# Re-timed steps in the attention plan of a fused attention and two-MLP kernel: natural keys of chunk 2, GpSimd's products of block 0, masks of chunk 5

## The chip, the cores and the metric

The kernel runs on one core of one Trainium2 chip. The metric is the device time of one execution in microseconds (us), lower is better. The kernel before takes 418.03 us, the median of 3 runs (417.99 to 418.68).

## The reference

Three layers follow one another, all in 32-bit floating point. Only the first and the routing part of the third matter for the change.

```python
# 1. attention with a decaying state: B, H, S, D = 2, 8, 768, 48
for t in range(S):
    cur = einsum('bhd,bhe->bhde', u * k[t], v[t])
    y[:, :, t] = einsum('bhd,bhde->bhe', r[t], state + cur)
    state = w * state + einsum('bhd,bhe->bhde', k[t], v[t])
# 2. x = y as 1536 tokens x 384; h = x @ w_in (384 x 2048); x2 = elu(h) @ w_out
# 3. logits = x2 @ w_gate (8 experts); expert = argmax; gate = softmax probability of it
#    each token takes the next of its expert's 384 places, goes through
#    relu(x2 @ w1[e]) @ w2[e], and comes back times its gate
```

## The kernel before

**Chunks, blocks, steps.** The 1536 tokens are 12 chunks of 128; six chunks make one batch element, and within it the attention state is carried from chunk to chunk. Two chunks make a block of 256 tokens for the first MLP, so there are six blocks (n = 0 to 5). A block has 16 steps (f = 0 to 15), one for each 128 of the 2048 hidden features. Steps are counted through: step q = 16 n + f, so block 0 is steps 0 to 15 and block 1 is steps 16 to 31. Chunks 0 and 1 are computed before step 0. The attention of chunks 2 to 11 is spread over the MLP's steps, as small pieces on each engine.

**A step on each engine.** Each product is made of three matmuls from a high and a low part of both operands.
- TensorE: fc1(f) (L1475), nine matmuls of 256 columns; then the attention pieces of the step; then, in block 1 and later, the routing's count (L1564) where it is due; then fc2 of three steps ago (L1501), six matmuls. fc1 of step q waits until VectorE has finished the elu of step q-2 (its PSUM bank is free then). fc2 of a step waits for that step's g_lo.
- ScalarE: in block 0 relu(-h) (L861), which waits for g_lo of step q-2, since that frees the elu buffer; exp (L863); a weight cast; the cast g_hi (L872).
- VectorE: from block 1 on min(h, 0) (L1179); the elu itself (L1187); and after it the step's attention pieces and the routing. In block 0 two weight splits of 128x384 a step (wd_lo, L1057 and L1062), one ahead of the elu and one behind it.
- GpSimd: g_lo = elu - g_hi (L707), then the step's attention pieces, by `ahead` (L687).

**The attention pieces of a chunk c.** GpSimd makes the decayed keys and queries (`keys` L638, `queries` L644), the bonus product r*k (`raw_bonus` L602) times u (`with_u` L611), the decayed natural keys (`natural_k1` L616, tile nat, 128x512), and the diagonal (`diagonal` L626, two selects). VectorE sums the bonus (`sum_bonus` L1015) and masks the scores in two halves (`mask` L1020). TensorE makes the scores (L1363), the outer product of natural keys and values (`outer` L1394, which waits for the natural keys), and the result (`back` L1411).

**What sets the order.** Every engine runs its own queue in order. `meeting(c)` and `plan(c)` (L330 to L354) say by hand in which step each piece of a chunk is issued: meeting is 2, 9, 17, 22 and 29 for chunks 2 to 6. An engine asks `chunk_for(what, n, f)` (L358) in every step. In `ahead` the diagonal comes first, then the decay, then natural keys, keys, queries, rk, with_u. On VectorE the masks stand ahead of the routing pieces of the same step.

With the kernel before, the pieces that the change speaks of stand as follows.
- GpSimd, block 0: step 2 diagonal(2) and decay; step 3 natural(2) and keys(3); step 4 queries(3); step 5 rk(3); step 6 with_u(3); step 7 diagonal(3); step 8 natural(3); step 9 nothing.
- VectorE: mask(2, second half) in step 7, ahead of the sum of chunk 3's bonus; mask(5) in steps 23 and 24.
- TensorE: outer(2) in step 9, behind scores(3) and ahead of back(2) and fc2 of step 6. outer(3) is in step 13.

**The routing of block 0's tokens** (`route(0)`, L319) runs in block 1 on VectorE: shift in step 23 (L1098: a copy of 128x8, a maximum, a subtraction), choose in step 24 (L1113: key L1115, maximum L1117, onehot L1118, the sum `before` L1119, n_seen L1121), gates in step 25 (L1123: a sum L1126, a scalar add L1127, a reciprocal L1128, a copy L1129, a product L1130, a sum L1131), place in step 27. Each operation waits for the one before it. TensorE's count of step 26 waits for L1119. On GpSimd steps 23 to 26 carry keys(6), queries(6), rk(6) and with_u(6).

```python
def fc1(n, f):
    q = FT * n + f
    wait_if(pe, s_g, q - 1)
...
def count(n):
    pe.wait_ge(s_round, 2)
    pe.wait_ge(s_oh, n + 1)
...
def outer(c):
    pe.wait_ge(s_k1n, n_states(c + 1))
```

Of the kernel before, what the change touches and what calls it, by code (L numbers as in the profile page):

```python
# [12 lines left out]
def build(nc, B, H, S, D, DFF, NE, FE, CAP, rkt_in, nat_in, decay, bonus, bonus_pair, win, wout, wouttr, wgate, wexp, out, slots):  # L13
# [163 lines left out]
    with ctx:  # L177
# [152 lines left out]
        def meeting(c):  # L330

            return {2: 2, 3: 9, 4: FT + 1, 5: FT + 6, 6: 2 * FT - 3}.get(c, 2 * FT + 3 + 8 * (c - 7))

        def plan(c):

            b, before = meeting(c), meeting(c - 1)
            steps = {"scores": b, "decay": b + (2 if c > 4 else 0), "keys": before + 1, "queries": before + 2,
                     "mask0": b + (c > 4), "mask1": b + 1 + (c > 4)}
            if c == 2:
                steps.update(diagonal=2, mask0=4, mask1=7, natural=3, outer=9, back=9, state=10, low=11)  # L340
                del steps["keys"], steps["queries"]
            elif c < 5:
                steps.update(rk=before + 3, with_u=before + 4, sum=before + 5, diagonal=before + 5, natural=before + 6)
                if c == 3:
                    steps.update(decay=12, outer=13, back=13, low=13, state=14)
            else:
                steps.update(rk=b - 2, with_u=b - 1, sum=b, diagonal=b, natural=b + 4)
            if c == 6:
                steps.update(rk=b - 4, with_u=b - 3)
            if c == 7:  # L350
                steps.update(rk=b - 3)
            if c > 3:
                steps.update(outer=meeting(c + 1), state=meeting(c + 1), back=meeting(c + 1), low=meeting(c + 1))
            return steps  # L354

        PLANS = {c: plan(c) for c in range(2, NSTEP)}

        def chunk_for(what, n, f):  # L358
# [1505 lines left out]
```

## Time and profile before

| | |
|---|---|
| median of 3 runs | 418.03 us (417.99 to 418.68) |
| the profiled execution | 418.21 us, its span 416.5 us |
| TensorE busy | 407.3 us, 98% |
| VectorE busy | 243.5 us, 58% |
| ScalarE busy | 188.0 us, 45% |
| GpSimd busy | 231.8 us, 56% |
| mean granted TensorE clock | 0.997 |

The span is what the profiler sees between the first and the last instruction; the time is 1.7 us longer. Engines in the rows below: PE is TensorE, PEld its weight loads, DVE VectorE, ACT ScalarE, POOL GpSimd. A row of a timeline gives the start in us from the span's start, the duration in us, the engine, the line, the operation, the tiles and the shapes. "x1" is one instruction. In square brackets stands how long the engine was idle before it and what ended that. Matmuls are pipelined: a 256-column matmul is shown with 0.28 us, and the next one starts 0.12 us later.

### The profile page before, as it was taken

The page shows a single profiled execution, that of the slowest core. Times are in us where ns is not written, and L with a number is a line of the kernel's source. Part 1 is how long each engine was busy: PE and PEld are TensorE (multiplying, and loading weights), DVE is VectorE, ACT ScalarE, POOL GpSimd, SP SyncE. Part 2 cuts the span into 40 slices and gives each one's busy share as a digit, 9 for nine tenths or more (in the row PEclk, how much of TensorE's full clock was granted, in tenths as well). Part 3 has the DMA queues.
Part 4 walks back from the last instruction along what each step waited for, and adds up shares of the span by engine and source line. Part 5 has one row for each costly group of instructions (what it writes and reads, how often), then busy time and mean ns, then how long its engine had stood idle before and what let it go on. Part 6 is the DMA issues. An engine that isn't in the chain of part 4 may idle for free.

```text
span 416.5 us, 9128 instructions
## 1 busy us (share of the span) xinstructions
PE 407.3 (98%) x3537; PEld 391.2 (94%) x3537; DVE 243.5 (58%) x576; ACT 188.0 (45%) x409; POOL 231.8 (56%) x239
## 2 busy tenths in 40 slices
PE   8999999999999999999999999999999999999994
PEld 7798799999999999999999999999999999999994
DVE  7788754376567546754663487785535545364521
ACT  4777453223433343334343455553646445574520
POOL 3789856557865786578334335166083562826531
PEclk9999999999999999999999999999999999999998
DMA  7998997123130403020009001826373835739000
GB/s 258 400 395 347 321 373 279 35 83 102 56 118 0 139 19 120 2 87 19 3 2 357 3 0 40 312 89 221 150 302 89 352 136 227 275 102 358 7 33 28
DMA packets 18649, 64.97 MB, mean 156 GB/s; under 512 B 2203, under 2 KB 11717, under 8 KB 16432
## 3 DMA queue, kind: packets, MB, share of 16 engines
q1 hardware_dynamic: 16816, 59.68, 39.2%
q0 software_dynamic: 1792, 4.73, 3.0%
q8 instruction: 27, 0.44, 0.4%
q14 instruction: 14, 0.11, 0.1%
HBM read 51.98 MB, written 13.21 MB: 157 GB/s over the span
## 4 chain that ended last, share of the span: by engine, by line
PE 90%; DVE 3%; POOL 2%; issue 2%; DMA 1%; ACT 0%; SPq 0%; POOLq 0%; DVEq 0%; ACTq 0%
PE bank L1359 26%; PE bank L1361 25%; PE bank L1360 25%; PE bank L1377 2%; DMA rkt<-rkt 1%; PE bank L1406 1%; PE bank L1442 1%; PE bank L1446 1%; PE bank L1680 1%; PE bank L1435 1%; POOL g_lo L707 1%; PE bank L1438 1%; DVE wd_lo L1057 1%; PE bank L1533 1%; PE bank L1715 1%
## 5 line engine op out<-in xcount | busy, mean ns | idle before, releaser
L707 POOL TENSOR_TENSOR g_lo<-elu,g_hi 128x256 fp32r<-128x256 f32 x95 | 73.7, 777 | 88.4 <-ACT g_hi L872 88.2
L1359 PE MATMUL bank<-xt,wd_hi 128*128 128x256 f32 x285 | 80.8, 284 | 0.5 <-DVE elu L1187 0.3
L1361 PE MATMUL bank<-xt,wd_lo 128*128 128x256 f32 x285 | 80.5, 282 | 0.0
L1360 PE MATMUL bank<-xt,wd_hi 128*128 128x256 f32 x285 | 80.4, 282 | 0.0
L863 ACT ACTIVATE elu<-elu 128x256 f32<-128x256 f32 x96 | 40.1, 418 | 77.0 <-DVE elu L1179 76.5
L1359 PE MATMUL bank<-wd_hi,g_hi 128*128 128x392 f32 (+1 forms) x192 | 67.6, 352 | 0.2 <-POOL g_lo L707 0.2
L1187 DVE SCALAR_TENSOR_TENSOR elu<-elu,bank 128x256 f32<-128x256 f32 x96 | 40.3, 419 | 43.7 <-ACT elu L863 43.7
L1361 PE MATMUL bank<-wd_hi,g_lo 128*128 128x392 f32 (+1 forms) x192 | 65.2, 340 | 0.0
L1360 PE MATMUL bank<-wd_lo,g_hi 128*128 128x392 f32 (+1 forms) x192 | 65.2, 339 | 0.0
L872 ACT CAST g_hi<-elu 128x256 fp32r<-128x256 f32 x96 | 39.0, 406 | 42.9 <-DVE elu L1187 42.9
L1359 PEld LDWEIGHTS bank<-xt,wd_hi 128*128 128x128 f32 x285 | 54.0, 189 | 1.6 <-DVE elu L1187 1.5
L1361 PEld LDWEIGHTS bank<-xt,wd_lo 128*128 128x128 f32 x285 | 54.2, 190 | 0.0
L1360 PEld LDWEIGHTS bank<-xt,wd_hi 128*128 128x128 f32 x285 | 54.0, 190 | 0.0
L1291 DVE SCALAR_TENSOR_TENSOR ge_lo<-bank,ge_hi 128x256 fp32r<-128x256 f32 x56 | 23.8, 424 | 48.8 <-ACT ge_hi L930 48.8
L1179 DVE TENSOR_SCALAR elu<-bank 128x256 f32<-128x256 f32 x80 | 33.8, 422 | 31.4 <-PE bank L1361 26.8
L930 ACT ACTIVATE ge_hi<-bank 128x256 fp32r<-128x256 f32 x56 | 21.6, 385 | 54.5 <-PE bank L1361 32.5
L724 POOL TENSOR_TENSOR wd_lo<-wd_raw,wd_hi 128x1024 fp32r<-128x1024 f32 x12 | 30.4, 2560 | 26.6 <-ACT wd_hi L943 24.2
L1359 PEld LDWEIGHTS bank<-wd_hi,g_hi 128*128 128x128 f32 x192 | 36.3, 189 | 3.4 <-issue 2.4
L1360 PEld LDWEIGHTS bank<-wd_lo,g_hi 128*128 128x128 f32 x192 | 36.5, 190 | 0.0
L724 POOL TENSOR_TENSOR we_lo<-we_raw,we_hi 128x1024 fp32r<-128x1024 f32 x9 | 21.3, 2398 | 27.1 <-ACT we_hi L943 27.1
L1361 PEld LDWEIGHTS bank<-wd_hi,g_lo 128*128 128x128 f32 x192 | 36.1, 188 | 0.0
L729 POOL DMA_INDIRECT out<-yrow,tok_i x16 | 15.7, 983 | 18.6 <-DVE yrow L1311 11.7
(220 smaller groups left out, 946.9 us busy)
## 6 DMA issues: line engine op xcount, KB each, us to landing
we_raw<-wexp SPq DMA_DIRECT2D x8, 1536.0 KB, 7.0
wd_raw<-wexp SPq DMA_DIRECT2D x8, 1536.0 KB, 6.7
rkt<-rkt SPq DMA_DIRECT2D x12, 512.0 KB, 5.6
nat<-nat SPq DMA_DIRECT2D x9, 672.0 KB, 4.3
xrow<-slots SPq DMA_DIRECT2D x16, 193.0 KB, 7.0
wd_raw<-win SPq DMA_DIRECT2D x4, 768.0 KB, 9.3
wd_raw<-wout SPq DMA_DIRECT2D x4, 768.0 KB, 9.5
wo_tr<-wouttr SPq DMA_DIRECT2D x1, 3072.0 KB, 18.6
```

The lines of the kernel that those rows point to most:

```text
L707: nc.gpsimd.tensor_tensor(g_lo[:, f % 4, :], elu[:, f % 2, :], g_hi[:, f % 4, :].bitcast(F32), ALU.subtract).then_inc(s_glo, 1)
L724: nc.gpsimd.tensor_tensor(EL[r][:, cols], ER[r][:, cols], EH[r][:, cols].bitcast(F32), ALU.subtract).then_inc(s_elo2[r], 1)
L729: nc.gpsimd.indirect_dma_start(out=out, out_offset=bass.IndirectOffsetOnAxis(ap=tok_i[r][:, t, :], axis=0), in_=yrow[r][:, t, :], in_offse ...
L863: nc.scalar.activation(elu[:, f % 2, :], elu[:, f % 2, :], ACT.Exp, scale=-1.0 if n == 0 else 1.0).then_inc(s_exp, 1)
L872: nc.scalar.copy(g_hi[:, f % 4, :], elu[:, f % 2, :]).then_inc(s_ghi, 1)
L930: nc.scalar.activation(ge_hi[:, f % 4, :], ps_e[f % 2][:, 0:SN], ACT.Relu).then_inc(s_gehi, 1)
L1179: V.tensor_scalar_min(elu[:, f % 2, :], ps_h[f % 2][:, 0:BN], 0.0).then_inc(s_m, 1)
L1187: V.scalar_tensor_tensor(out=elu[:, f % 2, :], in0=elu[:, f % 2, :], scalar=-1.0, in1=ps_h[f % 2][:, 0:BN], op0=ALU.add, op1=ALU.max).then ...
L1291: V.scalar_tensor_tensor(out=ge_lo[:, f % 4, :], in0=ps_e[f % 2][:, 0:SN], scalar=0.0, in1=ge_hi[:, f % 4, :].bitcast(F32), op0=ALU.max, o ...
L1359: mm(dst, w_hi, x_hi, start=start, stop=False)
L1360: mm(dst, w_hi, x_lo, start=False, stop=False)
L1361: return mm(dst, w_lo, x_hi, start=False, stop=stop)
```

## The change

Only the table in `plan` changes. Nothing is added or removed, and no wait condition is edited.
- Chunk 2: the second mask goes from step 7 to step 6, the natural keys from step 3 to step 7.
- Chunk 3: the diagonal goes from step 7 to step 8, the natural keys from step 8 to step 9.
- Chunk 5: the two masks go from steps 23 and 24 to steps 25 and 26. In step 25 the first one stands ahead of the gates.

```diff
             if c == 2:
-                steps.update(diagonal=2, mask0=4, mask1=7, natural=3, outer=9, back=9, state=10, low=11)
+                steps.update(diagonal=2, mask0=4, mask1=6, natural=7, outer=9, back=9, state=10, low=11)
                 del steps["keys"], steps["queries"]
             elif c < 5:
                 steps.update(rk=before + 3, with_u=before + 4, sum=before + 5, diagonal=before + 5, natural=before + 6)
                 if c == 3:
-                    steps.update(decay=12, outer=13, back=13, low=13, state=14)
+                    steps.update(diagonal=8, natural=9, decay=12, outer=13, back=13, low=13, state=14)
             else:
                 steps.update(rk=b - 2, with_u=b - 1, sum=b, diagonal=b, natural=b + 4)
+            if c == 5:
+                steps.update(mask0=b + 3, mask1=b + 4)
             if c == 6:
```

After it GpSimd's block 0 reads: step 3 keys(3), step 4 queries(3), step 5 rk(3), step 6 with_u(3), step 7 natural(2), step 8 diagonal(3), step 9 natural(3).

## Rows read from the trace of the kernel before

**Rows 1.** The page: chain by engine, granted TensorE clock in 40 slices.

```profile
PE 90%; DVE 3%; POOL 2%; issue 2%; DMA 1%; ACT 0%; SPq 0%; POOLq 0%; DVEq 0%; ACTq 0%
PEclk9999999999999999999999999999999999999998
```

**Rows 2.** Timeline of TensorE in block 0: start, us, engine, line, operation.

```profile
30.36 0.28 PE L1359 MATMUL bank<-xt,wd_hi 128*128 128x256 f32 x1
...
31.80 0.44 PE L1359 MATMUL bank<-wd_hi,g_hi 128*128 128x384 f32 x1 [0.21 <-POOL g_lo L707]
...
35.69 0.39 PE L1359 MATMUL bank<-xt,wd_hi 128*128 128x256 f32 x1
...
38.22 0.69 PE L1406 MATMUL bank<-nat 128*64 128x64 f32 x16
```

**Rows 3.** Timeline of GpSimd in block 0.

```profile
26.58 1.05 POOL L707 TENSOR_TENSOR g_lo<-elu,g_hi 128x256 fp32r<-128x256 f32 x1
27.59 1.69 POOL L624 TENSOR_TENSOR nat<-nat,pwn 128x512 f32<-128x512 f32 x1
29.24 1.50 POOL L642 TENSOR_TENSOR k<-rkt,powers 128x512 f32<-128x512 f32 x1
...
37.16 0.72 POOL L707 TENSOR_TENSOR g_lo<-elu,g_hi 128x256 fp32r<-128x256 f32 x1
```

**Rows 4.** Timeline of VectorE in block 0.

```profile
29.61 1.54 DVE L1057 TENSOR_TENSOR wd_lo<-wd_raw,wd_hi 128x384 fp32r<-128x384 f32 x1
```

**Rows 5.** Timeline of TensorE in block 1, steps 24 to 28.

```profile
85.09 0.28 PE L1361 MATMUL bank<-xt,wd_lo 128*128 128x256 f32 x1
...
89.38 0.28 PE L1361 MATMUL bank<-xt,wd_lo 128*128 128x256 f32 x1
90.28 0.25 PE L1573 MATMUL bank<-onehot,earlier_r 128*128 128x16 f32 x1 [0.62 <-issue]
...
91.68 0.38 PE L1359 MATMUL bank<-xt,wd_hi 128*128 128x256 f32 x1
...
93.92 0.33 PE L1359 MATMUL bank<-xt,wd_hi 128*128 128x256 f32 x1
```

**Rows 6.** Timeline of VectorE in block 1, steps 23 to 26.

```profile
84.52 0.75 DVE L1028 COPY_PREDICATED att<-earlier,bank 128x512 f32<-128x512 uint32 x1
85.15 0.74 DVE L1101 CAST before<-n_seen 128x8 fp32r<-128x8 f32 x1
...
86.23 0.42 DVE L1179 TENSOR_SCALAR elu<-bank 128x256 f32<-128x256 f32 x1
87.13 0.42 DVE L1187 SCALAR_TENSOR_TENSOR elu<-elu,bank 128x256 f32<-128x256 f32 x1 [0.48 <-ACT elu L863]
...
88.10 0.74 DVE L1115 SCALAR_TENSOR_TENSOR key<-lg,rank 128x16 f32<-128x16 f32 x1
...
89.08 0.91 DVE L1118 TENSOR_TENSOR onehot<-key,col 128x16 fp32r<-128x16 f32 x1
90.02 0.17 DVE L1119 TENSOR_TENSOR before<-before,onehot 128x8 fp32r<-128x8 f32 x1
...
91.21 0.42 DVE L1187 SCALAR_TENSOR_TENSOR elu<-elu,bank 128x256 f32<-128x256 f32 x1 [0.48 <-ACT elu L863]
...
91.74 0.17 DVE L1127 TENSOR_SCALAR col<-col 128x2 f32<-128x2 f32 x1
...
93.40 0.42 DVE L1187 SCALAR_TENSOR_TENSOR elu<-elu,bank 128x256 f32<-128x256 f32 x1 [0.48 <-ACT elu L863]
```

**Rows 7.** Timeline of GpSimd in block 1, steps 23 to 25.

```profile
85.83 1.20 POOL L642 TENSOR_TENSOR k<-rkt,powers 128x512 f32<-128x512 f32 x1
88.07 0.74 POOL L707 TENSOR_TENSOR g_lo<-elu,g_hi 128x256 fp32r<-128x256 f32 x1 [1.05 <-ACT g_hi L872]
88.77 1.19 POOL L648 TENSOR_TENSOR r<-rkt,powers 128x512 f32<-128x512 f32 x1
...
92.84 1.02 POOL L607 TENSOR_TENSOR rku<-nat 128x384 f32<-128x384 f32 x1
```

## Prediction

> **What bounds the kernel now.** I read the page's chain first: TensorE is 90% of it, at full granted clock in every slice but the last [rows 1]. A moved piece of GpSimd or VectorE is therefore worth only what TensorE waits for it. Next the waits of TensorE: they are few and short, so I went through its timeline for places where a step is too long. The undisturbed step is 2.14 us: the last matmuls of fc1 in steps 24 and 26 are 4.29 us apart [rows 5]. Two places stand out in the stretch that the change touches.
>
> Block 0: fc1 of steps 7 and 9 start 5.33 us apart where two steps are 4.28, so 1.05 us are lost. The row in between shows fc2 of step 4 released by GpSimd's g_lo [rows 2]. That g_lo is late because natural(2) and keys(3) lie ahead of it (1.69 and 1.50 us, [rows 3]).
>
> Block 1: the count of step 26 starts at 90.28, while the last matmul of fc1(26) starts at 89.38 and the next could follow 0.12 later, at 89.50. So 0.78 us are lost. What ended it is the sum L1119, done at 90.19 [rows 5, 6].
>
> **Whose turn it is between VectorE and GpSimd** decides this case. The copy L1101 of 8 columns takes 0.74 us at 85.15, until GpSimd has gone over to keys(6) at 85.83; L1115 takes 0.74 beside a g_lo of 0.74 that ends at 88.81; L1118 takes 0.91 beside queries(6), which ends at 89.96. L1119 and L1127, alone, take 0.17 [rows 6, 7]. So such a small operation, issued while a GpSimd product runs, ends 0.03 us after that product. It goes the other way too: keys took 1.50 us in block 0 with a weight split waiting beside it and 1.20 in block 1 without [rows 3, 4, 7]. I read that as 0.3 us added to a GpSimd product for each split that gets in ahead of it.
>
> **Part 1, block 0.** Removed from step 3: natural(2). g_lo(4) then ends some 1.6 us earlier, at about 30.2, and fc1(9) can start at 34.6 instead of 35.69. The 1.05 us are gone at this point. But natural(2) now stands behind g_lo(7), and outer(2), in step 9, waits for it. From g_lo(3) at 26.58 to the end of g_lo(7) at 37.88 GpSimd issues 10 instructions back to back [rows 3]. After the change the same ten are there in another order, natural(2) last. No order makes the sum smaller, so natural(2) ends at about 37.9 if as many splits get in between as before (6 by my reading). VectorE is early too and waits less, so I count one to one and a half more at 0.3: 38.2 to 38.35. Outer(2) started at 38.22 before [rows 2]. With 0.05 for the signal and 0.1 for a restart of TensorE it starts at 38.3 to 38.5. **Term: +0.2 us**; ends -0.3 (no further split in between) and +0.5 (two more). TensorE waits there about 1.2 us in one piece, with back(2) and fc2(6) queued behind.
>
> The rest of part 1 I cost at nothing. keys, queries, rk and with_u come 1 to 1.7 us sooner; their loads were issued before 23 us in an unchanged order, and nothing on SP waits for them. The sum of chunk 3's bonus comes sooner and frees VectorE. Diagonal(3), now in step 8, no longer waits for that sum. It ends near 41.2, and mask(3) behind it near 42, while TensorE wants that mask only at the gated product of step 12. natural(3) ends near 43.5, needed in step 13. The second mask of chunk 2 is an exchange of 0.63 us between two steps of VectorE; the room is there as long as relu waits for g_lo. If that cover went, fc1(9) would be late by up to that much, and outer(2) hides 1.2 us of it. No DMA moves.
>
> **Part 2, block 1.** All times up to fc1(26) on the clock of before.
> - Step 23: without the mask, 0.63 us (84.52 to 85.15), the shift starts at 84.52, ahead of g_lo(23), and is done by 85.1. min(24) now waits for fc1(24) only: 85.09 + 0.28 + 0.05 = 85.42, 0.81 earlier than 86.23. The elu follows 0.90 later, as in [rows 6]: 86.32.
> - Step 24: choose begins 0.34 behind it (0.97 less the mask), at 86.66. L1115 waits for keys(6), to 87.06. L1118 is issued at 87.3, just behind g_lo(24) at 87.26 (0.94 behind its elu, as 88.07 is behind 87.13), and ends at 88.03. L1119 meets queries(6), which starts 0.70 behind g_lo(24), at 87.96, and takes 1.19: it ends at 89.18. The count needs it at 89.5. **The wait of 0.78 is gone**, by a margin of 0.3 us.
> - Step 25: the elu starts 1.02 behind the end of L1119, as 91.21 behind 90.19: 90.20, done 90.62. TensorE reaches fc1(27) at 89.50 + 0.22 + 1.06 = 90.8 without a wait and wants fc1(28) at 92.9. fc1(28) needs the elu of step 26. Before, that elu started 2.19 behind the one of step 25. Now the mask adds 0.63, and the gates slide under GpSimd's work: L1127 would start at 90.20 + 0.53 + 0.63 = 91.36, inside g_lo(25) (91.14 to 91.88), and ends at 91.9. The reciprocal, the copy and the product behind it then meet rk(6), from 91.84 for 1.02 us [rows 7], and come through at 92.9. Before, the reciprocal ran at 91.94 and the elu of step 26 followed 1.46 later [rows 6]; now that is 92.8 + 1.46 = 94.2 to 94.3, done at 94.7.
> - So fc1(28) starts at 94.7 where it stood at 93.92 [rows 5]. TensorE gains 0.78 us at the count and waits 1.8 us two steps later. **Term: +0.8 us**; ends -0.4 (the gates slip through between two products, below) and +1.1 (one more product met).
> - Step 26: the second mask puts min(27) back by 0.63; its elu ends near 96.6, and fc1(29) wants it at 96.9. Place is done near 98.1, and back(5), which waits for it, comes at 99.2. scores(6) wants the masks at 98.1 and has them at 95.4. Nothing new, with 0.3 us to spare at the tightest.
>
> **Sum**: +0.2 + 0.8 = +1.0 us. The profiled execution took 418.21 us with a span of 416.5, so it would be 419.2 with 417.5. It stands 0.2 above the median, so against that: 418.03 + 1.0 = 419.0. From step 29 on TensorE has no gap that could take the loss back.
>
> **A rule against a term.** The gates' L1127 is one-source work of two elements, and my only one-source row is the copy L1101, of eight. The Trainium skill, "SBUF — State Buffer", section "Who interferes with whom", says that reductions never contend with GpSimd, that products with both inputs in SBUF do against its reads, and that copies and scalar forms do only when their operands meet the conditions of the two-port mode. By that page L1127 could run beside g_lo(25); what this would give is the first rival.
>
> **Rivals.**
> 1. *The gates slip between two products.* If L1127 isn't held by g_lo(25), it ends at 91.5, the reciprocal and copy by 91.7, and the product L1130 is asked for before rk(6) starts. It ends at 91.9, the elu of step 26 at about 93.5, and fc1(28) starts 0.4 earlier than before. With part 1's +0.2: -0.2, 417.8. For it: margins of 0.1 us. Against it: L1101 was held. Chance 0.16.
> 2. *Both waits go and nothing takes their place*: faster. Up to -0.8 in block 1, and part of the 1.05 in block 0: 416.1 to 417.3. Against it stand the unchanged sum of ten instructions ahead of outer(2), and 0.63 us of mask ahead of an elu with 0.1 us of slack (done 93.82, used 93.92). Chance 0.10.
> 3. *Half right*: block 1 as forecast, block 0 with fewer splits in between, -0.3 to -0.5: 418.4. Chance 0.12.
> 4. *The clock*: two idle stretches of 1.2 and 1.8 us might cost a lower granted clock, 2.1 us more for each step at half speed: 421 or more. Against it: the clock is full throughout [rows 1], with short waits only. Chance 0.04.
>
> The forecast has the remaining 0.58. The range, 417.4 to 419.8, holds it with its ends and rivals 1 and 3. A measurement of this kernel can tell about 0.2% (0.84 us) from no change, so slower begins at 418.87. The forecast lies just above that, and I put three quarters of it there: 0.43, with the clock 0.47. Faster is rival 2 and a little of rival 1: 0.12. The rest, 0.41, is same.
>
> **What would show it.** In the changed profile: no idle time at L1573; a wait of TensorE at L1406 of step 9 released by natural(2), about 1.2 us; a wait at fc1(28) released by VectorE's elu, 1.5 to 2 us; L1127 and L1128 or L1129 at 0.5 and 0.9 us. It would be wrong if natural(2) ends by 37.2, or if the gates' operations stay at 0.17 us.

## The result and the profile after

| | before | after |
|---|---|---|
| median | 418.34 us (20 runs) | 419.31 us (20 runs) |
| the profiled execution | 418.21 us | 419.95 us |
| its span | 416.5 us | 418.2 us |
| TensorE busy | 407.3 us | 407.2 us |

The ratio is 1.0023, with a 95% interval of 1.0016 to 1.0030: the kernel is 1.0 us slower (0.7 to 1.3). By the prediction's own bar of 0.2% that is slower, though the interval begins just below the bar. 419.0 was forecast against a median of 418.03. TensorE's busy time is the same, so the loss is idle time. The profiled execution is the longest of the 20 of its kernel. Its attention starts about 0.5 us late: the diagonal of chunk 2 runs at 24.73, against 24.19 before, ahead of anything that was moved. So I compare distances within a profile. The two inserted lines shift every later line number by 2.

TensorE's waits between 15 and 110 us, changed kernel (who waited, for whom, us in total, times, longest):

```profile
PE bank L1361 <- DVE elu L1189: 2.3, 2, 1.5
PE bank L1408 <- POOL nat L626: 1.0, 1, 1.0
```

The one-off wait at the count (L1573 before) is gone from the list. The 1.0 us at outer(2) and the 1.5 us at an fc1 are new. The rest of the 2.3 us is a wait of 0.87 us at an fc1 at 19.31. Before it was 0.30 there, as in all ten other kernels profiled below; it lies ahead of everything that was moved, so it belongs to this execution and not to the change. The timeline of TensorE shows where:

```profile
36.56 1.16 PE L1379 MATMUL bank<-r,k 64*128 64x128 f32 x16
...
38.73 0.69 PE L1408 MATMUL bank<-nat 128*64 128x64 f32 x16 [1.00 <-POOL nat L626]
...
90.04 0.17 PE L1575 MATMUL bank<-onehot,earlier_r 128*128 128x16 f32 x1
...
95.10 0.39 PE L1361 MATMUL bank<-xt,wd_hi 128*128 128x256 f32 x1 [1.47 <-DVE elu L1189]
...
98.51 1.16 PE L1379 MATMUL bank<-r,k 64*128 64x128 f32 x16
...
100.66 0.78 PE L1448 MATMUL bank<-att,nat 128*32 128x128 f32 x16
```

The count starts at 90.04 without idle time, where before it had 0.62 [rows 5]. From there to the fc1 of step 28 are 5.06 us; before, from 90.28 to 93.92, 3.64. VectorE shows why:

```profile
85.06 0.16 DVE L1103 CAST before<-n_seen 128x8 fp32r<-128x8 f32 x1
...
87.19 0.40 DVE L1117 SCALAR_TENSOR_TENSOR key<-lg,rank 128x16 f32<-128x16 f32 x1
...
87.83 0.73 DVE L1120 TENSOR_TENSOR onehot<-key,col 128x16 fp32r<-128x16 f32 x1
88.60 1.11 DVE L1121 TENSOR_TENSOR before<-before,onehot 128x8 fp32r<-128x8 f32 x1
...
90.74 0.42 DVE L1189 SCALAR_TENSOR_TENSOR elu<-elu,bank 128x256 f32<-128x256 f32 x1 [0.49 <-ACT elu L865]
91.08 0.74 DVE L1030 COPY_PREDICATED att<-earlier,bank 128x512 f32<-128x512 uint32 x1
91.70 0.17 DVE L1128 TENSOR_REDUCE col<-prob 128x2 f32<-128x16 f32 x1
91.90 0.54 DVE L1129 TENSOR_SCALAR col<-col 128x2 f32<-128x2 f32 x1
92.48 0.17 DVE L1130 RECIPROCAL x2row<-col 128x2 f32<-128x2 f32 x1
92.56 0.85 DVE L1131 COPY x2row<-tokens 128x2 f32<-128x2 f32 x1
...
94.63 0.42 DVE L1189 SCALAR_TENSOR_TENSOR elu<-elu,bank 128x256 f32<-128x256 f32 x1 [0.48 <-ACT elu L865]
```

GpSimd beside them, and its block 0:

```profile
27.12 0.73 POOL L709 TENSOR_TENSOR g_lo<-elu,g_hi 128x256 fp32r<-128x256 f32 x1
27.82 1.51 POOL L644 TENSOR_TENSOR k<-rkt,powers 128x512 f32<-128x512 f32 x1
29.28 1.06 POOL L709 TENSOR_TENSOR g_lo<-elu,g_hi 128x256 fp32r<-128x256 f32 x1
...
37.10 1.58 POOL L626 TENSOR_TENSOR nat<-nat,pwn 128x512 f32<-128x512 f32 x1
...
88.49 1.20 POOL L650 TENSOR_TENSOR r<-rkt,powers 128x512 f32<-128x512 f32 x1
91.68 0.74 POOL L709 TENSOR_TENSOR g_lo<-elu,g_hi 128x256 fp32r<-128x256 f32 x1 [1.99 <-ACT g_hi L874]
92.38 1.01 POOL L609 TENSOR_TENSOR rku<-nat 128x384 f32<-128x384 f32 x1
```

Read the two together. The scalar add of two elements, L1129, takes 0.54 us and ends at 92.44, as g_lo ends at 92.42. The copy L1131 takes 0.85 and ends at 93.41, as rk ends at 93.39. The mask ahead of them holds VectorE for 0.62 us. The elu of step 26 starts 3.89 us behind that of step 25, where before it was 2.19 [rows 6]. The three parts make up the difference of 1.70: 0.62 for the mask, 0.37 for the add (0.17 before), 0.70 for the copy (0.15 before).

### The profile page after: what moved, and what is told of

It is laid out like the page before. It is cut to its first block, busy times and chain, and to the rows that moved or that the text cites. A ratio compares the mean times of both kernels' runs of the same rounds, so it can differ in the third digit from the quotient of the medians.

```text
span 418.2 us, 9128 instructions
## 1 busy us (share of the span) xinstructions
PE 407.2 (97%) x3537; PEld 392.0 (94%) x3537; DVE 243.7 (58%) x576; ACT 188.4 (45%) x409; POOL 231.4 (55%) x239
## 4 chain that ended last, share of the span: by engine, by line
PE 84%; DMA 5%; DVE 3%; POOL 3%; issue 2%; ACT 1%; SPq 0%; POOLq 0%; DVEq 0%
PE bank L1361 25%; PE bank L1363 24%; PE bank L1362 24%; DMA wd_raw<-win 3%; DMA xrow<-slots 2%; PE bank L1379 2%; POOL g_lo L709 1%; PE bank L1408 1%; PE bank L1448 1%; PE bank L1444 1%; PE bank L1682 1%; PE bank L1437 1%; PE bank L1440 1%; PE bank L1535 1%; PE bank L1717 1%
```

## The experiments

All were timed in five rounds against the kernel before. Each edit stands against the kernel before, unless it says "changed".

**1 and 2: each half alone**

```diff
+            if c == 5:
+                steps.update(mask0=b + 3, mask1=b + 4)
```

> Only chunk 5's masks are moved to steps 25 and 26; block 0 is as before. Theory (the loss is in block 1: the mask and the gates together make the elu of step 26 late): slower than before by 0.6 to 0.9 us, no idle time at the count, and a wait of about 1.5 us at the fc1 of step 28, released by VectorE's elu. Rival (the loss sits in block 0, and the masks gain what the count waited for): faster than before by 0.5 to 0.8 us.

Measured: 419.23 us against 418.14, ratio 1.0030 (1.0018 to 1.0042), so 1.1 us slower (0.8 to 1.8) where 0.6 to 0.9 was expected. The profile has no wait at the count and one of 1.46 us at the fc1 of step 28. From the scores of step 22 to those of chunk 7, later in the kernel, it is 36.36 us where it was 35.52 before.

```diff
-                steps.update(diagonal=2, mask0=4, mask1=7, natural=3, outer=9, back=9, state=10, low=11)
+                steps.update(diagonal=2, mask0=4, mask1=6, natural=7, outer=9, back=9, state=10, low=11)
...
-                    steps.update(decay=12, outer=13, back=13, low=13, state=14)
+                    steps.update(diagonal=8, natural=9, decay=12, outer=13, back=13, low=13, state=14)
```

> Only block 0's part of the change; chunk 5's masks in steps 23 and 24 as before. Theory (the waits of steps 4 to 9 are gathered into one at outer(2), behind GpSimd's unchanged sum of work): within 0.3 us of before, with a wait of about 1 us at outer(2), released by natural(2). Rival (the waits of steps 4 to 9 are gone and block 0 is shorter): faster by 0.7 to 1.1 us. Second rival (extra blocking between the splits and GpSimd's products): slower by 0.3 to 0.5 us.

Measured: 418.32 against 418.14, ratio 1.0007 (0.9998 to 1.0016). TensorE's waits between 15 and 130 us:

```profile
PE bank L1406 <- POOL nat L624: 1.5, 1, 1.5
PE bank L1573 <- issue: 0.6, 1, 0.6
PE bank L1359 <- DVE elu L1187: 0.3, 1, 0.3
```

The gathered wait at outer(2) is there, 1.5 us, and block 0 ends 0.15 us later than it did (39.33 us from the diagonal of step 2 to the scores of step 17, where it was 39.18). The first rivals of both runs fall: the loss is the masks', but for that 0.15. The second rival of this run, 0.3 to 0.5 us slower, is not excluded by time, whose interval reaches 0.7 us; the profile speaks against it.

**3: is it GpSimd's work beside the gates, or the mask alone?** rk and with_u of chunk 6 one step later, first on the changed kernel, then on the one with the masks alone.

```diff
             if c == 6:
-                steps.update(rk=b - 4, with_u=b - 3)
+                steps.update(rk=b - 3, with_u=b - 2)
```

> The changed kernel, with GpSimd's product rk of chunk 6 in step 26 instead of 25 and with_u in 27 instead of 26, so that only g_lo of step 25 runs beside the gates. Theory (part of the wait at the fc1 of step 28 is the gates' operations held by rk(6)): the copy L1131 of the gates falls from 0.85 us to about 0.15, and the kernel is 0.6 to 0.8 us faster than the changed one, about as before (within 0.2 us). Rival (the mask's 0.63 us alone makes the elu late, the blocking is hidden): no difference to the changed kernel, 0.7 to 1.0 us slower than before.

Measured: 419.22 against 418.14, ratio 1.0025 (1.0014 to 1.0036): by time the rival, by its profile the theory. The copy took 0.15 us and the wait at fc1 was 0.78 instead of 1.47. The gain was lost again in back(5) of step 29. From scores(6) to the fc2 behind back(5) are 3.37 us here; it was 2.70 before (97.28 to 99.98) and 2.86 in the changed kernel. Timeline of TensorE in it:

```profile
97.67 1.16 PE L1379 MATMUL bank<-r,k 64*128 64x128 f32 x16
...
99.82 0.61 PE L1448 MATMUL bank<-att,nat 128*32 128x128 f32 x12
100.67 0.43 PE L1448 MATMUL bank<-att,nat 128*32 128x128 f32 x4 [0.24 <-issue]
101.04 0.45 PE L1361 MATMUL bank<-wd_hi,g_hi 128*128 128x392 f32 x1
```

The last four matmuls come late, with no wait in the code between them and the twelve ahead. So I repeated the test without the altered block 0.

> Block 0 as before, chunk 5's masks in steps 25 and 26 as in the change, and GpSimd's rk of chunk 6 in step 26, with_u in 27. It repeats the test of GpSimd's blocking without the altered block 0. Theory: the wait at the fc1 of step 28 is about 0.8 instead of 1.5 us. If the last matmuls of back(5) don't lose time, the kernel is 0.6 us faster than the one with the masks alone moved; if they again lose about 0.5 us, it is within 0.2 us of that one.

Measured: 418.33 against 418.24, ratio 1.0003 (0.9994 to 1.0012), where the masks alone gave 1.0030. The lag in back(5) did not appear (97.57 to 100.27, 2.70 us). VectorE in it:

```profile
91.65 0.55 DVE L1129 TENSOR_SCALAR col<-col 128x2 f32<-128x2 f32 x1
...
92.31 0.15 DVE L1131 COPY x2row<-tokens 128x2 f32<-128x2 f32 x1
...
93.68 0.42 DVE L1189 SCALAR_TENSOR_TENSOR elu<-elu,bank 128x256 f32<-128x256 f32 x1 [0.48 <-ACT elu L865]
```

The add is held by g_lo as in the changed kernel; the copy, with rk away, is not. The elu of step 26 follows that of step 25 after 3.19 us instead of 3.89, so that one product of GpSimd is 0.7 us of the path. From the scores of step 22 to those of chunk 7 it is 35.51 us, as before the change and 0.85 less than with the masks alone: 0.70 is the product, 0.15 the lag in back(5), which that kernel had (below) and this one has not.

**4: where the masks should stand**

```diff
+            if c == 5:
+                steps.update(mask0=b + 4, mask1=b + 6)
```

(on the changed kernel, in place of its b + 3 and b + 4)

> The change, with chunk 5's masks in steps 26 and 28 instead of 25 and 26, so that neither shares a step with shift, choose, gates or place. Theory (the count's wait of 0.78 us goes, and the elu of step 26 is on time once no mask stands ahead of the gates): 1.4 to 1.7 us faster than the changed kernel, 0.6 to 0.9 us faster than before, with no wait at the fc1 of step 28. Rival (the count waits for something else as well, or the masks merely move the wait to the scores of step 29): no faster than before.

Measured: 420.08 against 418.14, ratio 1.0057 (1.0044 to 1.0070). A miss, and my own: the gates ran free (the elu of step 26 2.19 us behind that of step 25, no wait at fc1), but in step 28 the second mask is later than TensorE wants it.

```profile
98.25 1.16 PE L1379 MATMUL bank<-r,k 64*128 64x128 f32 x16 [1.82 <-DVE att L1030]
```

In this plan TensorE runs one step ahead of VectorE's elu: the mask that VectorE issued in step 28 was done at 98.10, and the scores of step 29 waited for it. So the masks in steps 26 and 27, with block 0 as before:

> Block 0 as before; chunk 5's masks in steps 26 and 27. Theory (the loss of the change came from the mask ahead of the gates, and that of the masks in 26 and 28 from the second mask coming after TensorE wanted the scores of step 29): neither the count, nor the fc1 of step 28, nor the scores of step 29 waits; faster than before by 0.6 to 0.9 us. Rival (place of step 27 is now late and back(5) waits for it, or the last matmuls of back(5) lose 0.2 to 0.6 us as they did in the kernels with masks moved): between 0.4 us faster and no faster.

Measured: 417.32 against 418.07, ratio 0.9982 (0.9974 to 0.9991), 0.75 us faster, with no wait at any of the three places. The theory holds. From the scores of step 22 to those of chunk 7 it is 34.52 us, 1.00 less than before.

**5: does block 0 have the 1.05 us to give?**

```diff
-                steps.update(diagonal=2, mask0=4, mask1=7, natural=3, outer=9, back=9, state=10, low=11)
+                steps.update(diagonal=2, mask0=4, mask1=7, natural=5, outer=9, back=9, state=10, low=11)
...
-                    steps.update(decay=12, outer=13, back=13, low=13, state=14)
+                    steps.update(rk=6, with_u=7, sum=8, natural=8, diagonal=9, mask0=10, mask1=11, decay=12, outer=13, back=13, low=13, state=14)
```

> Block 0 in another order, chunk 5's masks as before. GpSimd: natural(2) in step 5, rk(3) in 6, with_u(3) in 7, natural(3) in 8, diagonal(3) in 9, chunk 3's sum in step 8 and its masks in steps 10 and 11. So only six instead of ten of GpSimd's instructions stand ahead of outer(2) after g_lo(3). Theory (block 0 is bound by how much GpSimd work stands ahead of what TensorE waits for): the waits of steps 4 to 9 go and none comes at outer(2), faster than before by 0.8 to 1.1 us. Rival (TensorE's gated product of step 12 then waits for chunk 3's second mask, or VectorE's splits become the bound): no faster than before, with a new wait at L1533 or at an fc1.

Measured: 420.17 against 418.07, ratio 1.0055 (1.0042 to 1.0068). Outer(2) starts without a wait at 37.17 (38.22 before), and the gain is lost at the gated product:

```profile
47.68 2.78 PE L1533 MATMUL bank<-wo_tr,gate_w 128*32 128x512 f32 x24 [1.66 <-DVE att L1028]
```

The rival, then, and the same mistake of mine once more: a mask in VectorE's step 11, wanted in TensorE's step 12. With both masks of chunk 3 in step 10 (`mask1=10`):

> As the kernel with natural(2) in step 5, but with both masks of chunk 3 in step 10. Theory (what ate the gain there was the gated product of step 12 waiting for a mask issued behind the elu of step 11): VectorE finishes both masks near 44.9 us, TensorE wants them near 45.8, so that wait goes and 1.0 us is left: 0.8 to 1.1 us faster than before, and no drop of the granted clock. Rival (VectorE's step 10 gets too long and the elu or a split becomes late): a new wait at an fc1 of steps 11 to 13, no faster than before.

Measured: 416.78 against 418.24, ratio 0.9964 (0.9952 to 0.9976), 1.5 us faster: more than forecast. TensorE starts the gated product at 45.98 with no wait. From the diagonal of step 2 to the scores of step 17 it takes 37.85 us (24.53 to 62.38) where it was 39.18. That is 1.33 us, more than the 1.05 read from steps 7 to 9. Another 0.56 came in block 1, where nothing was edited (19.21 us from the scores of step 22 to those of step 29, 19.77 before): see the last section. The diagonal of step 2 itself ran 0.34 us later than before in this execution.

**6: both together**

> The last two together: GpSimd's other order in block 0, and chunk 5's masks in steps 26 and 27. Theory (two independent waits of TensorE, each worth its own length): the two gains add up, 1.4 to 2.0 us faster than before. Rival (the gain of one is given back at the other or later): no faster than the better one alone.

Measured, with chunk 3's second mask still in step 11: 417.94, ratio 1.0002 (0.9991 to 1.0012). This is the rival. The masks' gain is there (18.78 us between the scores of steps 22 and 29, 19.77 before). Block 0's is not: 39.84 us to the scores of step 17 instead of 39.18, with a wait of 1.95 us at the gated product.

> The same block 0, with chunk 5's masks in steps 26 and 27. Theory (each wait of TensorE is worth its length, and they add up): 1.6 to 2.0 us faster than before, 416.1 to 416.5 us. Rival (something in between absorbs the second gain): no faster than the better of the two alone.

Measured, with both of them in step 10: 415.82 against 418.24, ratio 0.9940 (0.9926 to 0.9953). At 2.4 us faster (2.0 to 3.1) it beats both kernels, and the 1.6 to 2.0 expected. By the profile block 0 gives 1.32 us and the stretch between the scores of steps 22 and 29 gives 0.99. Of TensorE's waits between 15 and 130 us one group is left:

```profile
PE bank L1361 <- DVE elu L1189: 0.3, 1, 0.3
```

## Why the prediction was right

**Block 0, term +0.2.** The waits of steps 4 to 9 did become one at outer(2): 1.0 us in the changed kernel, 1.5 with this half alone, where about 1.2 was forecast. The ten instructions from g_lo(3) to the end of natural(2) took 11.56 us (27.12 to 38.68) where the ten of before took 11.30 [rows 3]. I had expected 0.3 to 0.45 more and got 0.26. From the diagonal of step 2 to the scores of step 17 the changed kernel takes 39.17 us (24.73 to 63.90) and the one before 39.18. In the profiles of the half alone and of two other kernels with the same block 0 it is 39.33 to 39.36. So the term lies between 0.0 and +0.2, at or below what I put there.

**Block 1, term +0.8.** The chain came out as worked up to the copy, on a clock shifted by 0.54. L1119 of before ended at 89.71 (forecast 89.72), the elu of step 25 started at 90.74 (90.74), the scalar add ended at 92.44 (92.44), the copy at 93.41 (93.44). The elu of step 26 started at 94.63 instead of 94.74 to 94.84, and its fc1 at 95.10 instead of 95.24. The reason is a detail that I had wrong: the reciprocal, 0.17 us at 92.48 while rk ran, is not held by GpSimd; the copy behind it is. I had counted the 1.46 us to the elu from a held reciprocal. It starts 1.22 us after the end of the copy in both kernels.

Two smaller things did not come out. TensorE's wait at the fc1 of step 28 is 1.47 us in the profile, or 1.63 from the moment its queue was free (93.47: the last matmul of fc2 starts at 93.29 and the next would follow 0.18 later), where 1.8 was forecast. And the wait at the count had cost more than the 0.78 read there: from the count to the fc1 of step 28 are 3.64 us before and 3.43 in the changed kernel until its queue was free. So the 0.78 and the 1.8 of the prediction do not subtract to its +0.8. The term did not suffer, since it was taken from the starts of that fc1: by them 0.78 was forecast and 0.64 came (95.10 less the shift of 0.54, against 93.92).

From the scores of step 22 to those of step 29 the changed kernel takes 0.69 us more than before (20.46 against 19.77); up to the scores of chunk 7 it is 0.81 (36.33 against 35.52). The rows of the scores, three before (L1377) and three changed (L1379):

```profile
77.51 1.16 PE L1377 MATMUL bank<-r,k 64*128 64x128 f32 x16
...
97.28 1.16 PE L1377 MATMUL bank<-r,k 64*128 64x128 f32 x16
...
113.03 1.16 PE L1377 MATMUL bank<-r,k 64*128 64x128 f32 x16
```

```profile
78.05 1.16 PE L1379 MATMUL bank<-r,k 64*128 64x128 f32 x16
...
98.51 1.16 PE L1379 MATMUL bank<-r,k 64*128 64x128 f32 x16
...
114.38 1.16 PE L1379 MATMUL bank<-r,k 64*128 64x128 f32 x16
```

Only the 0.69 is the chain that I worked out. The rest comes behind the chain (the last paragraph of this section), so that the total meets the forecast to 0.03 us is in part luck.

**The rule against a term.** The Trainium skill, "SBUF — State Buffer", section "Who interferes with whom", lets scalar forms contend with GpSimd when their operands meet the two-port conditions, and does not say that two elements fail them. I had taken it for a reason why the two-element add could run beside g_lo. The trace decides against that reading, not against the section: the add took 0.54 us in the changed kernel and ended with g_lo. What the Trainium skill says there of reductions (never held) agrees with the sum L1128 of the changed kernel, 0.17 us inside g_lo's 91.68 to 92.42.

**The rivals.** The gates did not slip through. Both waits went, but others took their places, as argued. The clock did not fall in the changed kernel: the mean granted clock was 0.996 to 1.000 in all 20 runs.

**What was not in the sum.** In the changed kernel the last matmuls of back(5) take 0.16 us more (100.66, 0.78 us, where it was 0.62). It is within the range and was not foreseen. Its cause stays open. It was 0.15 with the masks alone, 0.37 with the masks in steps 26 and 28, 0.67 in the first rk run and nothing in the second. A lag of about 0.1 us stands there with block 0's half alone as well, where no mask was moved, so the masks' steps are not its condition. No row shows what the matmuls waited for.

## What to carry to other kernels

A wait removed from the bounding engine is worth its length only if every queue behind it is as far ahead; add up the work that stands before the next thing the engine wants, for moving work inside that sum gains nothing. In this kernel TensorE runs a step ahead, and a mask that it wants in step q had to be issued two steps earlier (step 27 for 29, step 10 for 12); one step earlier was too late both times. And a chain of tiny dependent operations on VectorE can cost the rest of a GpSimd product at each link: here the copy, the add and the products with two operands in SBUF were held for 0.2 to 0.9 us beyond their own length, the sums and the reciprocal were not. Look first at which long product stands in its step: moving one was worth 0.7 us.

## What the runs showed that I had not expected

**A tie decides 0.6 us.** In the kernel with both of chunk 3's masks in step 10, the time lost at the count fell from 0.78 to 0.21 us (the last matmul of fc1 at 88.39, the count at 88.72) although block 1 is unedited. Before, g_lo of step 23 started 0.02 us ahead of the copy L1101, and the copy took 0.74 us [rows 6]:

```profile
85.13 0.74 POOL L707 TENSOR_TENSOR g_lo<-elu,g_hi 128x256 fp32r<-128x256 f32 x1 [5.01 <-ACT g_hi L872]
```

In that kernel g_lo again starts 0.02 us ahead of it, and the copy isn't held:

```profile
84.16 0.16 DVE L1101 CAST before<-n_seen 128x8 fp32r<-128x8 f32 x1
```

```profile
84.14 0.77 POOL L707 TENSOR_TENSOR g_lo<-elu,g_hi 128x256 fp32r<-128x256 f32 x1 [5.00 <-ACT g_hi L872]
```

Here GpSimd's g_lo took 0.03 us longer instead. With block 0's half alone and with natural(2) in step 5 the copy is held as before, again 0.02 or 0.03 us behind g_lo. The recorded starts don't show who comes first in such a tie; what tips it was not tried, and with one profile of each kernel nothing shows whether it falls the same way in every execution.

**Lower clocks were seen only in the kernels with the longest waits.** In the kernel with the masks in 26 and 28 (a wait of 1.82 us) and the one with a wait of 1.66 us at the gated product, the mean granted clock was 0.993 or 0.994 in 6 of 11 runs, and these took 419.9 to 421.2 us; the others took 419.3 to 420.1. In the first kernel with both halves rearranged (a wait of 1.95 us at the gated product) two runs of 12 had 0.994 and took 419.4; the other ten took 417.6 to 418.1. In the kernel with 1.66 us this lifts the median (420.17) above the profiled run (419.33): four of its five runs had the lower clock. With the masks in 26 and 28 it does not explain the median: the two middle runs, 420.06 and 420.09, had 0.997, and what made them 0.7 us longer than the profiled one (419.40) is not known. In the changed kernel, with 1.47 us, it never fell below 0.996. That the waits are the cause is argued from this, not tested; the profiled runs of the three kernels had such a wait and a mean of 0.999 or 1.000, so the wait alone does not bring the lower clock.
